# Host-laid inputs, V as the stationary operand, and a new order of the opening in an attention and two-MLP kernel

## What is computed

```python
k_sum = k.reshape(B, H, nb, block, D).max(axis=3)          # block = 32, nb = 24
v_sum = v.reshape(B, H, nb, block, D).mean(axis=3)
scores_l = scale * np.matmul(q, k.transpose(0, 1, 3, 2))   # kept where |i - j| < 16
scores_s = scale * np.einsum('bhsd,bhnd->bhsn', q, k_sum) + np.log(block)
a = softmax(concat(masked scores_l, scores_s))
x = np.matmul(a, concat(v, v_sum))                         # heads side by side: 1536 x 512
xn = x / sqrt(mean(x * x) + 1e-6) * rms_g
x = (silu(xn @ w_gate) * (xn @ w_val)) @ w_out             # 512 -> 1536 -> 512
out = (s * relu(x @ w_in) ** 2 + b) @ w_out2               # 512 -> 2048 -> 512
```

## Time and profile before

| | before |
|---|---|
| median of the runs | 690.12 us |
| the profiled execution | 691.99 us |
| its span on the core | 690.3 us |
| TensorE matmul busy | 669.2 us (97%) |
| VectorE busy | 381.7 us (55%) |
| ScalarE busy | 209.9 us (30%) |
| GpSimd busy | 155.8 us (23%) |

### The profile page before, as it was taken

How to read it: one execution, slowest core, us unless ns; L and a number is a source line. 1 busy time by engine, 2 the same in 40 slices (tenths; PEclk the granted TensorE clock), 3 DMA queues, 4 the chain that set the end, 5 groups by cost and what they waited for, 6 DMA issues and landing times.

```text
span 690.3 us, 9126 instructions
## 1 busy us (share of the span) xinstructions
PE 669.2 (97%) x3400; PEld 558.7 (81%) x3400; DVE 381.7 (55%) x649; ACT 209.9 (30%) x491; POOL 155.8 (23%) x180
## 2 busy tenths in 40 slices
PE   6989999799999999999999999999999999999998
PEld 6879978577888888887887888888888888888886
DVE  5665567954448752256666346772155664277520
ACT  4655535232324410144343313430022220044200
POOL 5321231313332111112221132211121212222210
PEclk9979999989999999999999999999999999999999
DMA  7827541332432233534232242324343224333201
GB/s 218 221 47 221 132 107 47 92 80 82 121 91 93 92 123 108 153 79 99 68 86 68 87 123 75 108 90 124 97 137 103 70 68 138 96 91 109 101 1 61
DMA packets 124506, 70.84 MB, mean 103 GB/s; under 512 B 32944, under 2 KB 115888, under 8 KB 124464
## 3 DMA queue, kind: packets, MB, share of 16 engines
q1 hardware_dynamic: 122736, 67.13, 34.1%
q10 hardware_dynamic: 1728, 3.15, 1.2%
HBM read 67.11 MB, written 3.15 MB: 102 GB/s over the span
## 4 chain that ended last, share of the span: by engine, by line
PE 92%; DVE 3%; issue 2%; DMA 1%; ACT 1%; SPq 1%; POOL 0%; DVEq 0%; POOLq 0%; ACTq 0%
PE mlp L368 20%; PE mlp L370 20%; PE mlp L369 20%; PE scores L496 3%; PE scores L495 3%; PE scores L497 3%; PE attn_out L355 3%; PE scores L336 2%; PE turns L343 2%; PE attn_out L352 2%; PE attn_out L496 2%; PE turns L496 2%; PE attn_out L495 2%; PE turns L495 2%; PE attn_out L497 2%
## 5 line engine op out<-in xcount | busy, mean ns | idle before, releaser
L1190 POOL TENSOR_SCALAR w_hi<-w_raw 128x1024 fp32r<-128x1024 f32 x108 | 124.6, 1154 | 348.0 <-PE mlp L370 251.8
L368 PE MATMUL mlp<-x_hi,w_hi 128*128 128x512 f32 (+1 forms) x512 | 199.0, 389 | 0.0
L369 PE MATMUL mlp<-x_lo,w_hi 128*128 128x512 f32 (+1 forms) x512 | 193.4, 378 | 0.0
L370 PE MATMUL mlp<-x_hi,w_lo 128*128 128x512 f32 (+1 forms) x512 | 193.4, 378 | 0.0
L843 DVE TENSOR_TENSOR w_lo<-w_raw,w_hi 128x1024 fp32r<-128x1024 f32 x108 | 138.1, 1281 | 68.2 <-POOL w_hi L1190 68.1
L368 PEld LDWEIGHTS mlp<-x_hi,w_hi 128*128 128x128 f32 x512 | 96.9, 189 | 19.5 <-issue 2.9
L370 PEld LDWEIGHTS mlp<-x_hi,w_lo 128*128 128x128 f32 x512 | 96.8, 189 | 18.1
L369 PEld LDWEIGHTS mlp<-x_lo,w_hi 128*128 128x128 f32 x512 | 97.0, 190 | 16.3
L944 DVE SCALAR_TENSOR_TENSOR elem<-elem,s_col 128x512 f32<-128x512 f32 x48 | 43.4, 909 | 34.6 <-ACT elem L705 34.6
L368 PE MATMUL mlp<-hid_hi,w_hi 128*128 128x512 f32 x144 | 58.3, 405 | 0.0
L370 PE MATMUL mlp<-hid_hi,w_lo 128*128 128x512 f32 x144 | 56.3, 391 | 0.0
(11 more groups left out here) (123 smaller groups left out, 874.0 us busy)
## 6 DMA issues: line engine op xcount, KB each, us to landing
w_raw<-in_moe_w_in SPq DMA_DIRECT2D x48, 256.0 KB, 3.0
w_raw<-in_moe_w_out SPq DMA_DIRECT2D x48, 256.0 KB, 2.9
w_raw<-in_moe_w_gate SPq DMA_DIRECT2D x36, 256.0 KB, 3.1
w_raw<-in_moe_w_val SPq DMA_DIRECT2D x36, 256.0 KB, 3.4
w_raw<-in_moe_w_out SPq DMA_DIRECT2D x48, 192.0 KB, 2.7
kv_tok<-in_k SPq DMA_DIRECT2D x8, 384.0 KB, 6.1
q_rows<-in_q SPq DMA_DIRECT2D x12, 256.0 KB, 3.5
kv_tok<-in_v SPq DMA_DIRECT2D x8, 384.0 KB, 5.3
```

Source lines behind the costliest of these rows:

```text
L368: pe.matmul(acc, wh, hi, start=first, stop=False)
L369: pe.matmul(acc, wh, lo, start=False, stop=False)
L370: return pe.matmul(acc, wl, hi, start=False, stop=final)
L1190: pool.tensor_scalar(w_hi[n % RING][:, :, :], w_raw[n % RING][:, :, :], 1.0, 0.0, ALU.mult, ALU.add).then_inc(w_hi_ready, 1)
```

## The change

The host lays the inputs out before the launch (`laid_out`). q arrives feature-first, one block per tile, and is loaded directly into `qT`, of which there are now three buffers. k arrives feature-first with padding and is loaded directly into `kT`. Weights arrive in blocks, so that one DMA with a long row per partition fills a slot, where there were two with rows of 512 bytes or more. V arrives in three layouts: token rows of batch 0 for its block sums, feature-first for batch 1, and padded windows for the products.

So `turn_q`, `order_k`, `turn_k` and the copies behind them are gone. V becomes the stationary operand of `pv` and the turned probabilities the moving one, so x comes out feature-first in PSUM and `turn_x` is gone. In the new `pv` the 64-feature halves of two heads go to the two halves of the output partitions. Since tokens now lie along the free axis, two things move. The division by the row sums is done on the probabilities before they are turned, by GpSimd (`normalise`, eight operations per tile). And the mean square needs a sum across partitions: ScalarE squares, VectorE adds the four blocks (`sum_squares`), TensorE multiplies by a matrix of ones (`mean_squares`), VectorE adds 1e-6 to a 128x128 tile (`add_eps`), GpSimd raises 128x128 elements to -0.5 (`inverse_rms`), and VectorE scales in four operations (`scale_x`). Score columns shrink from 192 to 184, the `pT` buffers become four, `pv` is one call per tile and waits for all four.

The block sums of V of batch 0 are six 512-column fp32 matmuls (`mean_v_rows`). Those of batch 1 are four reductions on VectorE (`sum_v`, steps 12 to 15) and four transposes on TensorE at step 36 (`turn_v_sums`), which waits for tile 5's x. The bases of the tiles, the steps of a tile, and the orders of the opening on every engine are new. The weight DMAs of slots 0 to 3 and the small constants are still issued by SyncE in the opening, in a new order.

The core of the diff (the constants, what TensorE does, the new helpers, and of TensorE's opening the new order alone):

```diff
+    S_AT, M_AT, E_AT = (0, 2), (0, 1, 2, 3), (1, 2, 3, 4)
+    I_AT, N_AT, T_AT, PV_AT = (3, 5), (3, 4, 5, 6), (5, 6, 7, 8), 10
+    SQ_AT, RED_AT, ONES_AT, XN_AT, HI_AT, LO_AT = 10, 11, 12, 12, 14, 15
+
+    BASES = ((8, 22, 39, 55), (2, 20, 38, 55), ())
+    K_AT = (28, 29, 30, 31)
+    VSUM_AT, V_TURN_AT = (12, 13, 14, 15), 36
...
+                sp.dma_start(kT[:, j, :], k_t[b, :, j * SP:(j + 1) * SP]).then_inc(k_loaded[j], 16)
+            def load_q(tau):
+                after(sp, scores_ready, 2 * (tau - 2))
+                sp.dma_start(qT[tau % 3][:, :, :].rearrange("p j n -> p (j n)"), q_t[tau]).then_inc(q_loaded[tau % 3], 16)
+
+            def load_rows(i):
+                cols = slice(2 * i * DM, 2 * (i + 1) * DM)
+                sp.dma_start(v_all[:, cols], v_rows[:, cols]).then_inc(rows_loaded[i], 16)
+
+            def load_v_t():
+                sp.wait_ge(v_summed, 1)
+                sp.dma_start(v_all[:, :], v_t[:, :]).then_inc(v_t_loaded, 16)
...
+            def mean_v_rows(i, bank):
+                pe.wait_ge(rows_loaded[i], 16)
+                for g in (2 * i, 2 * i + 1):
+                    last = pe.matmul(bank[:, :], means[:, g, :], v_all[:, g * DM:(g + 1) * DM],
                                     start=(g == 0), stop=(g == G - 1))
...
+            def turn_v_sums():
+                pe.wait_ge(v_sums_ready, 1)
+                pe.wait_ge(xn_ready, PER_B)
+                for j in range(NPAIR):
+                    last = pe.transpose(O[:, j * P:(j + 1) * P], v_sums[:, j, :], ident[:, :])
...
-            def turn_q(tau, bank):
-                pe.wait_ge(q_loaded, 16 * (tau + 1))
-                for j in range(NPAIR):
-                    last = pe.transpose(bank[:, j * P:(j + 1) * P], q_rows[:, j * P:(j + 1) * P], ident[:, :])
-                last.then_inc(q_turned, 1)
-
...
+                elif g == 0:
+                    pe.wait_ge(k_win_ready, windows_until(tau))
+                    pe.wait_ge(sums_ready, NPAIR * (tau // PER_B + 1))
...
+                        last = pe.matmul(banks[e][:, c0:c0 + KW], qT[tau % 3][rows, j, :], k_win[rows, j, 0:KW],
+                                         start=True, stop=True)
...
+                pe.wait_ge(normed, NPAIR * tau + j + 1)
+                both = probs[:, j, :, :].rearrange("p e n -> p (e n)")
...
+            def pv(tau):
+                buf, bank = tau % 2, out_bank(tau)
+                pe.wait_ge(v_loaded[buf], 64 * (tau // 2 + 1))
+                pe.wait_ge(v_sums_placed[0], tau // PER_B + 1)
+                pe.wait_ge(v_sums_placed[1], tau // PER_B + 1)
+                after(pe, xn_ready, tau if tau != 1 else 0)
+                pe.wait_ge(pT_even, 2 * tau + 2)
+                pe.wait_ge(pT_odd, 2 * tau + 2)
+                for j in range(NPAIR):
+                    pe.matmul(bank[:, j * P:(j + 1) * P], v_b[buf][:, j, :, :].rearrange("p e d -> p (e d)"), pT[j][:, 1, :],
+                              start=(j == 0), stop=False)
+                for j in range(NPAIR):
+                    for e in range(2):
+                        last = pe.matmul(bank[e * D:(e + 1) * D, j * P:(j + 1) * P], v_a[buf][:, e, j, :], pT[j][:, 2 * e, :],
+                                         start=False, stop=(j == NPAIR - 1))
                 last.then_inc(pv_done, 1)
 
-            def turn_x(tau, bank):
-                pe.wait_ge(xn_ready, tau + 1)
-                xr = x_rows[:, :, :].rearrange("p h d -> p (h d)")
-                for j in range(NPAIR):
...
+                        if g == 0 and tau % TILES == 0 and c > 0:
+                            pe.wait_ge(rows_dve, 2 * c)
+                            pe.wait_ge(rows_act, 2 * c)
                         pe.wait_ge(masked, NPAIR * tau + 2 * g)
...
+                for tau in at_step(c, s, ONES_AT):
+                    mean_squares(tau)
...
+                for tau in at_step(c, s, PV_AT):
+                    pv(tau)
+                if c == 0 and s == V_TURN_AT:
+                    turn_v_sums()
...
+            def mean_squares(tau):
+                pe.wait_ge(sq_summed, tau + 1)
+                after(pe, eps_added, tau)
+                pe.wait_ge(masked, NPAIR * (2 if tau < 2 else 4 if tau < TILES else tau + 1))
+                pe.matmul(mean_sq(tau), ones[:, :], sq_sum[:, :], start=True, stop=True).then_inc(meansq_ready, 1)
...
+                        pe.wait_ge(eps_added, 2)
+                    if n == 4:
+                        pe.wait_ge(xn_ready, 2)
...
+            early_scores(0, 1)
             pe.wait_ge(setup_done, MEANS)
+            mean_v_rows(0, M[3])
+            early_scores(1, 0)
+            mean_v_rows(1, M[3])
             early_turn(0, 0)
             early_turn(0, 1)
+            mean_v_rows(2, M[3])
             early_turn(0, 2)
             early_turn(0, 3)
             early_scores(1, 1)
+            pv(0)
             early_turn(1, 0)
             early_turn(1, 1)
             early_scores(2, 0)
             early_turn(1, 2)
             early_turn(1, 3)
+            mean_squares(0)
+            pv(1)
             early_scores(2, 1)
+            mean_squares(1)
             early_turn(2, 0)
+            early_scores(3, 0)
             early_turn(2, 1)
+            early_quarters(0, 1)
             early_turn(2, 2)
+            early_scores(3, 1)
             early_turn(2, 3)
+            early_quarters(1, 3)
+            pv(2)
             early_turn(3, 0)
+            early_quarters(3, 5)
             early_turn(3, 1)
+            mean_squares(2)
+            early_quarters(5, 6)
             early_turn(3, 2)
+            early_quarters(6, 8)
             early_turn(3, 3)
+            early_quarters(8, 10)
+            pv(3)
+            early_quarters(10, 13)
+            mean_squares(3)
+            early_quarters(13, 16)
             for c in range(NC):
                 stage1(c)
                 stage2(c)
@@ -623,62 +523,39 @@
 
         @block.scalar
         def _(act):
...
             def square_x(tau):
+                act.wait_ge(pv_done, tau + 1)
+                after(act, sq_summed, tau)
+                act.activation(squares[:, :, :], out_bank(tau)[:, :].rearrange("p (j n) -> p j n", j=NPAIR),
+                               ACT.Square).then_inc(squared, 1)
+
+            def x_high(tau):
+                act.wait_ge(xn_ready, tau + 1)
                 t = tau % TILES
...
+                after(dve, scores_ready, 2 * PER_B * b)
+                dve.tensor_reduce(k_win[:, j, LW:KW], kT[:, j, WINDOW:WINDOW + S].rearrange("p (n k) -> p n k", k=BLOCK),
+                                  AX_X, ALU.max).then_inc(sums_ready, 1)
+
+            def sum_v(j):
+                if j == 0:
+                    dve.wait_ge(v_t_loaded, 16)
+                    dve.wait_ge(setup_done, SETUP)
+                dve.tensor_reduce(v_sums[:, j, EVEN_SUMS:EVEN_SUMS + NB],
+                                  v_all[:, j * S:(j + 1) * S].rearrange("p (n k) -> p n k", k=BLOCK),
+                                  AX_X, ALU.add).then_inc(v_sum_ready, 1)
+
+            def invert_sums(tau, g):
+                n, heads = 2 * tau + g + 1, slice(4 * g, 4 * g + 4)
+                dve.wait_ge(exp_done, 2 * n)
+                after(dve, normed, NPAIR * (tau - 1) + 2 * g + 2)
+                dve.tensor_scalar(row_inv[:, heads], row_sum[:, heads], 1e-9, None, ALU.add).then_inc(rowsum_fixed, 1)
+                dve.wait_ge(rowsum_fixed, n)
+                dve.reciprocal(row_inv[:, heads], row_inv[:, heads]).then_inc(rowinv_ready, 1)
...
+            def sum_squares(tau):
+                dve.wait_ge(squared, tau + 1)
+                after(dve, meansq_ready, tau)
+                dve.tensor_reduce(sq_sum[:, :], squares[:, :, :].rearrange("p j n -> p n j"), AX_X,
+                                  ALU.add).then_inc(sq_summed, 1)
+
+            def add_eps(tau):
                 dve.wait_ge(meansq_ready, tau + 1)
+                after(dve, xn_ready, tau)
+                dve.tensor_scalar(rstd[:, :], mean_sq(tau), 1e-6, None, ALU.add).then_inc(eps_added, 1)
+
+            def scale_x(tau):
+                dve.wait_ge(rstd_ready, tau + 1)
+                after(dve, x1_hi_ready, tau)
+                after(dve, x1_lo_ready, tau)
...
+                for j in range(KC):
+                    last = dve.scalar_tensor_tensor(out=xn[:, j, :], in0=out_bank(tau)[:, j * P:(j + 1) * P],
+                                                    scalar=g_col[:, j:j + 1], in1=rstd[:, :], op0=ALU.mult, op1=ALU.mult)
+                last.then_inc(xn_ready, 1)
...
+            def normalise(tau, j):
+                pool.wait_ge(rowinv_ready, 2 * tau + j // 2 + 1)
+                for e in range(2):
+                    h, p_h = 2 * j + e, probs[:, j, e, 0:KW]
+                    last = pool.tensor_scalar(p_h, p_h, row_inv[:, h:h + 1], 0.0, ALU.mult, ALU.add)
+                last.then_inc(normed, 1)
 
             def inverse_rms(tau):
...
```

(49 more changed lines are left out.)

786 lines of the change are left out of this document (256 added, 530 removed).

## The result

The changed kernel takes 911.66 us (median of four runs, 910.41 to 912.34) against 690.83 for the kernel before in the same session: a ratio of 1.3195, interval 1.3165 to 1.3226. The prediction was 667.6, with 653 to 682 as its range. It was wrong in sign and far outside. Rival (b), "the power is dear", is what happened, at a price no row of before had shown.

What follows compares the result with a forecast made beforehand. TensorE, busy 669.2 of 690.3 us, was taken as the bound. Tiles 8.6, K's turns 2.8, V's means 6.1 and opening 5.0 sum to 22.5 us off, 667.6 against the median; 8-in-10 range 653 to 682.

Steps and rivals of the forecast that it cites:

- Rival (b): GpSimd's power is dear, slower than before: gain gone at X = 6.5, 706.6 us at X = 8; chance 0.10.
- X, the power: Time of the 128x128 power on GpSimd: taken as 3 us, bounds 0.8 and 39, called the largest unknown.
- The cover of 5 us per tile: Chunks 0 and 1: TensorE needs what waits behind `scale_x` later, so a 3 us power is hidden, 8 us not.
- The price of a tile: TensorE's time per attention tile in chunks 0 and 1: 1.1 us less, 8.6 us for eight tiles.
- in pairs, 0.11 apart: Sign in `pv`: passes writing different output halves start two at a time, 0.11 us apart, if the forecast is right.
- rival (a): Output halves in `pv` don't overlap, so 16 passes take 1.7 or 2.56 us: 674.6 or 681 us; chance 0.25.
- K's turns and V's means: Chunk 0, batch 1: dropping K's transposes gains 2.8 us, replacing V's small mean matmuls gains 6.1 us net.
- The wait at step 36: Chunk 0: TensorE's transposes of V's sums wait 2.8 us for tile 5's x, with X = 3.
- The opening: Before chunk 0's stage 1: first quarter at 43.2 us, end at 63.6 instead of 68.6; gain 5.0, bounds -1 and 11.
- the wait for `b_col`: Opening: VectorE's 3.08 us wait goes, as its DMA no longer stands behind loads waiting for two tiles: -3.1 us.
- The credit of 3 for the clock: Opening: of 4.7 us that TensorE lost at half clock between 38 and 48 us, 3 were credited as gained.
- At nothing: Fewer, larger weight DMAs, the fourth `pT` buffer, the single `pv` wait and GpSimd's divisions per tile: counted as zero.

Runs made afterwards that it cites:

- e8_sixteen: The changed kernel with its power on 16 of the 128 columns only: 691.9 us, ratio 1.0012 to the kernel before.
- e1_mult: The changed kernel with its 128x128 power replaced by a multiplication, so no inverse root is computed: 675.6 us, ratio 0.9777 to the kernel before.
- e5_cols: The changed kernel with a one-column power spread by a second ones matmul, and small scale-column transfers issued earlier in the opening: 682.0 us.
- e7_order: e5_cols with the opening's queues reordered, tile 3's sums one quarter earlier: 676.9 us, ratio 0.9816 to the kernel before.
- e9_weights: The kernel before with only the weight blocks laid out by the host, one transfer per slot instead of two: 688.7 us, ratio 0.9979.

## Why the prediction was wrong, step by step

**X, the power: the step that failed.** Taken 3 us, measured 20.8. The row it rested on was right, 0.703 for one column against 0.398 for a plain operation, and so were both bounds: 0.8 and 39. I chose near the low end on the ground that the extra 0.305 us "must hold a second operand and the start of a routine, which come once". No row said so. The runs show 0.16 us per column and 0.46 us of start-up, little over the 0.398 of a plain operation: about half of the extra recurs with every column. By the section's own break-even, X = 6.5, the sign hung on this one number, and with bounds of 0.8 and 39 around it (b) deserved far more than 0.10, and the range an upper end far above 682. Rival (b)'s formula 3(X - 3) + 8(X - 5) gives 180 us at 20.8, that is 847 us; measured were 912, since the opening has four powers in series and not two, and the cover is less than 5.

**The cover of 5 us per tile.** This is the rest of that miss. "TensorE comes a piece later" looked only at `silu` and `h_low`. The timelines show two other things in VectorE's queue behind `scale_x`: the next tile's masks, which free the banks for TensorE's scores, and x2's low part, which opens the next stage. At X = 3 the power is 2.4 us longer than the multiplication. Chunk 1 hides 2.2 of that, and pays 1.0 us for four tiles. Chunk 0 pays 10.6, more than four such powers are longer: by the trace about 5 us are waits and about 6 low clock behind them (an estimate, from the waits and the granted clocks of the two traces). The cover there was in part real, but the sum had no term for the clock that TensorE loses behind each wait that isn't covered. With X = 3 (e8_sixteen) the time is 691.9 and not 667.6: 10.5 us are missing in the opening (74.1 for 63.6), 11.9 in chunk 0 (130.6 for 131.9 - 13.2), 1.1 in chunk 1.

**The price of a tile: right.** In e1_mult chunk 1's stages 1 and 2 take 83.6 + 39.6 = 123.2 us for the 123.1 forecast; a tile costs (123.2 - 97.9) / 4 = 6.3 instead of 7.4 us, so 1.05 less for the 1.1. Its parts: 16 passes in 1.02 us for 0.88 + 0.2. The check "in pairs, 0.11 apart" is met, and rival (a) falls. GpSimd's divisions measure 542 ns for my 530 and cost TensorE waits of 1.1 us in chunk 0 and 0.5 in chunk 1 of e1_mult, nearly nothing as taken.

**K's turns and V's means.** With the multiplication chunk 0 gained 11.9 us. With so short a power the sum would be 4.3 + 2.8 + 8.6 = 15.7. The loss of clock behind the V means is gone, as forecast (the row of e1_mult there: clock 1.00):

```profile
68.40:75.40 7.00, 6.98 (x46) 6.99 (x47) 2.41 (x6) 1.60 (x4) 1.05 (x1) 0.76 0.00 0
...
131.00:143.00 12.00, 12.00 (x61) 9.57 (x62) 8.69 (x28) 6.20 (x21) 5.51 (x10) 1.00 0.14 36
```

The first row shows part of the 3.8 us that are missing: the stage now begins at 0.76, 7.0 x 0.24 = 1.7 us lost. A second stretch loses as much, 4.5 x 0.38 = 1.7:

```profile
86.00:90.50 4.50, 4.03 (x17) 3.80 (x18) 4.50 (x9) 0.54 (x2) 2.04 (x4) 0.62 0.36 117
```

It stands behind the first of two waits of TensorE in stages 1 and 2 for VectorE's copies of turned probabilities (view of the waits: us in total, times, longest):

```profile
PE turns L295 <- DVE pT L745: 2.7, 2, 1.6
```

Waits and clock together are more than the 3.8 us, so something else must have gained more than I counted; no run separates that. The wait at step 36, forecast at 2.8 with X = 3, is 2.24 in e8_sixteen and 20.1 in the changed kernel. Full clock behind it, which the prediction also forecast, did not come: it is the stretch at 0.57 from 137 us above.

```profile
137.39 0.95 PE L271 MATMUL attn_out<-ident,v_sums 128*128 128x128 f32 x4 [2.24 <-DVE xn L765]
```

**The opening: wrong even with a free power.** With X = 0.5 my terms put the first quarter at 38.2 and the end at 58.6; e1_mult has 45.1 and 68.4. What the terms had right: the first scores at 6.3 (6.6 forecast). What they had wrong: the wait for `b_col` did not go, and its removal is worth 1.1 us of the 3.1 I had credited (e5_cols). The credit of 3 for the clock: TensorE is granted 0.72 from 36 to 48 us in e1_mult still, and is busy for 6.7 us of these 12. And they were a list of savings taken off the old end, where the new path is a chain of its own: squares, sum (1.02 us), ones, root, scale (1.12), high and low part of tile 1. I never wrote that chain down from its start. Behind the first quarter I counted TensorE's work plus 1.5 us of waits, 20.4; it is 23.3, with 2.8 us of idle VectorE at 62.4 before tile 3's sum, which stands behind `times_value` in its queue, and 1.9 us of TensorE at the end:

```profile
62.44 0.42 DVE L787 SCALAR_TENSOR_TENSOR elem<-elem,mlp 128x256 f32<-128x256 f32 x1 [2.78 <-PE mlp L325]
62.78 1.02 DVE L750 TENSOR_REDUCE sq_sum<-squares 128x128 f32<-128x512 f32 x1
...
67.67 0.69 DVE L772 TENSOR_TENSOR x_lo<-xn,x_hi 128x512 fp32r<-128x512 f32 x1 [0.69 <-ACT x_hi L558]
```

Moving that sum one place forward is part of e7_order. How much of the 9.8 us is clock and how much chain no run separates.

**At nothing.** The weights' transfers: right to about 1 us, by e9_weights. Chunk 2 is unchanged to 0.1 us, as forecast.

## What to carry to other kernels

When an operation gets wider, its cost per column is the first thing to settle: two rows of different width give it, one row never does, and where bounds lie 0.8 to 39 us apart the chances must follow the bounds. Before a statistic is moved with its layout, ask which axis it will lie on, and keep roots and powers at one value per partition even if that takes a diagonal and a second matmul. Where TensorE's waits are counted, look at the granted clock behind each: it can cost as much again. And before a difference of 2 us is put down to an edit, compare executions of the same mean clock. An opening is predicted by writing the new chain from its first instruction, queue by queue, not by taking savings off the old end.
